# A routed expert stage on one core: ScalarE splits the next expert's weights ahead of a transposing transfer, and second-layer pieces ahead of the rows out

## The reference

```python
logits = x @ w_gate                       # 1792 tokens, 8 experts
e_idx = np.argmax(logits, axis=1)
...
for e in range(E):                        # w1[e] is 768 x 1024, w2[e] is 1024 x 768
    mask = e_idx == e
    ...
    h = np.maximum(x[mask] @ w1[e], 0.0)
    ye = h @ w2[e]
    out[mask] = gate_w[mask, None] * eom[mask, e, None] * ye
```

## Time and profile before

| | |
|---|---|
| median of 3 runs | 1074.93 us (1073.94 to 1076.77) |
| profiled execution | 1075.34 us, span of its trace 1073.5 us |
| PE busy | 1044.1 us, 97% of the span |
| DVE, ACT, POOL busy | 551.5, 422.8, 254.8 us |
| loads issued by SP and ACT for weights, queue q1 | 106.37 MB |
| granted TensorE clock | mean 0.998 of full |

### The profile page before, as it was taken

One profiled execution on the slowest core, in us unless ns is written; L12 is line 12 of the kernel. 1 busy time (PEld: TensorE's weight loads), 2 busy tenths in 40 slices (PEclk: granted clock), 3 DMA queues, 4 the chain that ended last, 5 costly groups with the idle time before them and its releaser, 6 DMA issues. The chain is left out here.

```text
span 1073.5 us, 20362 instructions
## 1 busy us (share of the span) xinstructions
PE 1044.1 (97%) x7916; PEld 608.4 (57%) x7916; DVE 551.5 (51%) x812; ACT 422.8 (39%) x610; POOL 254.8 (24%) x217
## 2 busy tenths in 40 slices
PE   7999999999999999999999999999999999998997
PEld 3434334434555555555555555556777877877775
DVE  7899999984434443333333321003547347256461
ACT  6788888886211111111111221001135335335441
POOL 5887778841000000000000100000112212212221
PEclk9999999999999999999999999999999999999999
DMA  6266877541411111111100432100399388388752
GB/s 159 62 139 138 171 149 158 125 96 36 133 50 51 49 51 55 58 59 59 59 30 1 161 104 74 44 29 30 103 245 297 98 271 274 103 274 262 235 152 48
DMA packets 145832, 125.91 MB, mean 117 GB/s; under 512 B 99825, under 2 KB 121711, under 8 KB 145761
## 3 DMA queue, kind: packets, MB, share of 16 engines
q1 hardware_dynamic: 113952, 106.37, 34.4%
q10 hardware_dynamic: 28640, 7.55, 4.7%
q0 software_dynamic: 3168, 11.02, 2.9%
HBM read 99.49 MB, written 13.85 MB: 106 GB/s over the span
## 5 line engine op out<-in xcount | busy, mean ns | idle before, releaser
L1722 PE MATMUL ps<-arena 128*128 128x448 f16 x1728 | 328.8, 352 | 0.0
L1722 PEld LDWEIGHTS ps<-arena 128*128 128x128 f16 x1728 | 168.2, 98 | 156.1 <-issue 0.5
L1737 PE MATMUL ps<-arena 128*128 128x392 f16 (+1 forms) x996 | 165.3, 329 | 0.0
L1290 DVE SCALAR_TENSOR_TENSOR arena<-arena 128x768 f16<-128x768 f32 (+1 forms) x112 | 112.7, 1067 | 101.3 <-ACT arena L983 100.5
L1801 PE MATMUL ps<-arena 128*128 128x384 f16 x864 | 144.4, 326 | 11.0 <-DVE arena L1510 10.9
L1793 PE MATMUL ps<-arena 128*128 128x128 f16 x2592 | 147.7, 219 | 0.0
L1793 PEld LDWEIGHTS ps<-arena 128*128 128x128 f16 x2592 | 146.2, 98 | 2.4 <-DVE arena L1493 0.2
L1737 PEld LDWEIGHTS ps<-arena 128*128 (+1 forms) x996 | 97.3, 98 | 66.9
L950 ACT ACTIVATE arena<-ps 128x448 f32<-128x448 f32 x48 | 26.1, 543 | 258.2 <-PE ps L1722 258.2
L1618 PE MATMUL ps<-arena 128*128 128x448 f32 x288 | 126.6, 562 | 0.0
L1801 PEld LDWEIGHTS ps<-arena 128*128 128x128 f16 x864 | 83.0, 98 | 67.2 <-DVE arena L1510 14.4
(11 more groups left out here) (183 smaller groups left out, 928.0 us busy)
## 6 DMA issues: line engine op xcount, KB each, us to landing
arena<-in_moe_w SPq DMA_DIRECT2D x48, 512.0 KB, 6.3
arena<-in_moe_w SPq DMA_DIRECT2D x64, 384.0 KB, 4.4
arena<-in_qk SPq DMA_DIRECT2D x23, 448.0 KB, 4.7
y_parts<-arena SPq DMA_DIRECT2D x16, 384.0 KB, 2.3
arena<-sums_inv SPq DMA_DIRECT2D x48, 112.0 KB, 2.9
arena<-in_v SPq DMA_DIRECT2D x24, 192.0 KB, 3.0
arena<-in_moe_w_gate SPq DMA_DIRECT2D x12, 384.0 KB, 4.1
arena<-in_moe_w_val SPq DMA_DIRECT2D x12, 384.0 KB, 5.5
```

Of the source, the lines that this page charges most:

```text
L1290: nc.vector.scalar_tensor_tensor(lo, raw_rows(e, p), S_OP, hi, ALU.mult, ALU.subtract).then_inc(w_lo_ready, 1)
L1722: last = nc.tensor.matmul(ps[:, 2 * (b % 2) + g, 0:S], up_w[s][:, g, c, wl], xt[:, b * KC + c, xl], start=(c == 0 and wl + xl == 0), stop= ...
L1737: last = nc.tensor.matmul(ps[:, 4 + 2 * s + h, 0:cols], gt[:, f, gl, bass.ds(t * 128, 128)], wo[:, f, wl, h, 0:cols], start=(f == 0 and gl ...
```

## The change

ScalarE's program alone is written in another order, inside the tile of the expert stage. In the opener of experts 1 to 7 the first four second-layer pieces are split ahead of `rows_done`, and in the opener of experts 1 to 6 the six pieces of the next expert are split ahead of `move_rows(g + 2)`. Tile 0 and all tiles that are not openers keep their order. No instruction is added or taken away, and no other engine's program changes.

```diff
             def tile(e, s, before, first):
                 g = before + 1
-                if not is_at(g, 0):
+                if is_at(g, 0):
+                    split_high(e, s, range(KC + 5, PIECES))
+                else:
+                    if first:
+                        split_high(e, s, range(KC, KC + 4))
                     rows_done(before)
-                if first:
-                    split_high(e, s, range(KC + 5, PIECES) if is_at(g, 0) else range(KC, KC + 4))
                 hidden(g, 0)
                 if first and not is_at(g, 0):
                     split_high(e, s, range(KC + 4, PIECES))
                 hidden(g, 1)
-                move_rows(g + 2)
+                if is_at(g, 0):
+                    move_rows(2)
                 if first and not is_at(e, E - 1):
                     split_high(e + 1, 1 - s, range(KC))
+                if not is_at(g, 0):
+                    move_rows(g + 2)
```

## The result

| | before | changed |
|---|---|---|
| median | 1074.43 us (4 runs) | 1088.77 us (4 runs, 1083.50 to 1089.43) |
| ratio, 95% interval | | 1.0114 (1.0080 to 1.0149) |
| profiled execution, its span | 1075.34, 1073.5 | 1083.50, 1081.6 |
| TensorE's waits from 790 us on | 10.9 | 16.4 |
| granted clock, mean | 0.998 | 0.993 |

The change made the kernel slower; forecast was 1066.5, so the blind prediction was wrong in sign. Its trace shows the kind of loss, and 8.1 us of it in the span.

The account below looks back on a forecast made before the run. TensorE, busy 97% of the span, was taken as the bound, with 10.9 us of expert-stage waits to win. Of these 8.9 could go, less 0.5: 8.4 off 1075.34 gives 1066.9, set at 1066.5 for the median; range 1064.8 to 1071.0.

Parts of the forecast that it names:

- I take 7.1, the nearest case: Transposing transfer moved behind six splits: 7.1 us from issue to landing beside loads, chosen among 5.9, 7.1 and 10.2.
- Not before its old time: GpSimd's gather of the next expert's opener rows, waiting for the transfer: expected 0.8 to 1.5 us before its old time.
- rival D: Slower, chance 0.08: transfer takes 10.2 us or more beside second-layer loads; four openers wait 2.7 each; 1.9 slower, 1076.8.
- D's point of decision: Transfer time from which the slower outcome, late gathers and waiting openers, was to decide: 9.7 us.
- The rule of packets: Transfer engines alternate between queues packet by packet: adds up to 12.5 us, transfer 15.7, kernel some 1099; held at 0.01.
- The first edit's gain in openers: Rows out behind four splits: VectorE's low half comes 0.8 to 0.9 us earlier; expert 1's opener keeps 0.2 + 0.4.
- The second's in followers: Six splits ahead of the transfer: waits for VectorE in four followers, 4.7 us in all, can go.
- ScalarE's path: ScalarE in followers, from the end of the transfer's issue to the next rows out: 0.6 us.
- the sum: TensorE's 10.9 us of expert-stage waits: 8.9 can go, less 0.5 for near misses, 8.4 gained; forecast 1066.5.

Follow-up runs that it names:

- number 3: Changed kernel, with SyncE holding loads of pieces 7 to 13 of experts 2 to 7 until the preceding opener's transposing transfer lands: 1069.33 us, ratio 0.9946.
- number 6: Changed kernel, loading only 384 of 768 columns of pieces 7 to 13 of experts 2 to 7 (output not the reference's): 1064.34 us, ratio 0.9897.
- number 9: Changed kernel, loading only 576 of 768 columns of pieces 7 to 13 of experts 2 to 7 (output not the reference's): 1069.27 us, ratio 0.9959.
- number 4: Kernel before, rows out still first, but two of the six next-expert splits ahead of the transposing transfer and four behind it: 1078.23 us, ratio 1.0039.
- number 1: Kernel before, with only the rows out moved behind four splits; the transposing transfer stays ahead of the six splits: 1078.57 us, ratio 1.0042.
- number 2: Kernel before, with only the transposing transfer moved behind the six splits; rows out stay first: 1093.49 us, ratio 1.0174.
- number 5: Kernel before, ScalarE's order unchanged, only loads of pieces 7 to 13 of experts 2 to 7 held until the transposing transfer lands: 1083.64 us, ratio 1.0060.
- number 7: Kernel before, two of six splits ahead of the transposing transfer, rows out first, second-layer loads held until that transfer lands: 1076.18 us, ratio 1.0015.

## Why the prediction was wrong

**The step that failed is one term:** "I take 7.1, the nearest case", the transfer's time beside loads. It took 11.7 to 12.7 us in the chain. I had priced it by transfers that ran beside first-layer loads, and hardly beside them: of the 7.1 us only 3.8 had packets of the transfer (1017.7 to 1021.5), with 112 load packets next to them, where expert 4's after had 9.2 us (949.7 to 958.9) and 331. The edit put it behind the six splits, and the low splits are what releases second-layer loads; so the edit both moved the transfer and queued up to six loads of 384 KB beside it. With them held it took 3.7 us, and the kernel 1069.3 (number 3). Numbers 3, 6 and 9 show that it is the load bytes beside it.

**"Not before its old time" became the bound.** I had the next gather at 0.8 to 1.5 us earlier than before, hidden by a few tenths. With 12 instead of 7 us it waited 7 to 10 us for the transfer, as rival D said. D's mechanism, place and direction are what happened; I gave it 0.08, and its price, 1.9 us slower against the 14.3 measured, was too low. It had a wait of 2.7 us in each of four openers; three waited 2.2, 4.1 and 3.8 us, and the fourth, expert 3's, 1.4 behind a stop of 2.5. And it left out that a long wait also slows the matmuls behind it: three groups at 9.65 instead of 7.97, 5.0 us. D's point of decision, 9.7 us of transfer, was about right: number 9's 10.1 us in expert 4 was followed by a wait of 0.28 in expert 5's opener, the changed kernel's 12.1 by one of 2.22.

**The rule of packets** (the Trainium skill, "DMA: Bandwidth & Descriptors", "Queues, rings and completion order") had given 15.7 us. The measured 12.4, and 15.9 in number 4, lie nearer to it than my 7.1. But my 15.7 took one load packet for each packet of the transfer, 1568, and beside expert 4's there were 331. The same section speaks of packets that typically hold some 9 to 17 descriptors, and no run here shows what the profile counts as a packet in these terms. So the nearness of 15.7 is in part luck. That halving the bytes of each load packet at about the same count took the transfer from 12.1 to 7.2 fits turns taken by packets; it doesn't exclude other ways of sharing. I had read two short rows against it, from a place where the queued loads were others.

**What was right.** The first edit's gain in openers: expert 1's waits fell from 1.5 to 0.2 us (0.6 forecast), and they were 0.4 in number 1 and 1.4 in number 2, which lacks this edit. The second's in followers: all four waits for VectorE are gone in the changed kernel. ScalarE's path: 0.5 us between the issue's end and the rows out in expert 4 (946.88 + 2.17 to 949.51), 0.6 forecast. Number 6 shows that with lighter loads the sum held: 1064.3 against 1066.5.

**What else was missed.** That each edit alone costs was not asked: the first one +4 (number 1), the second +19 (number 2). Together they cost 14 by the medians, and under the hold the first is worth 7.7. I had valued it at about 3 us. A part of why is traced above, the share of each part isn't measured.

**Open.** Of six executions of the changed kernel four took 1088.2 to 1089.4 and two, one of them the profiled, 1083.2 and 1083.5; what the four lose beyond that isn't seen. Number 5's loss by the hold is seen at one place only, and why number 7 gained so little is not settled.

## What to carry to other kernels

Before a transfer is moved behind work, ask what that work releases onto the same queues, and price the transfer among those neighbours, not among the ones it had. A buffer of one (`x_rows` here) turns the landing time of one transfer into the start of the next; find the step at which it decides and what it costs beyond the wait. If a reorder fails so, holding back the loads that are not yet needed can save it, but only together with it: the hold alone cost 6 us by its ratio here (9 by the medians), in part because the held loads then ran beside the next gather.

## What the runs showed of the hardware

**The clock after a wait.** Mean granted clock after, in the group behind the 2.2 us wait (973.40 to 983.00), and in an undisturbed one (955.20 to 963.10); columns: stretch, length, busy time and count of PE, PEld, DVE, ACT, POOL, then PEclk, DMA share, GB/s:

```profile
973.40:983.00 9.60, 9.51 (x49) 5.31 (x50) 9.45 (x12) 6.38 (x8) 3.55 (x4) 0.82 0.94 358
```

```profile
955.20:963.10 7.90, 7.90 (x54) 4.79 (x52) 1.68 (x3) 0.60 (x1) 1.08 (x2) 1.00 0.77 168
```

A mean of 0.82 over 9.6 us is some 3.5 us at the lower of the two levels (1.2 GHz), which costs 1.7 us, what the group was longer by. So the three long waits of this execution cost 1.7 us each beyond their length. It is not a matter of the length alone: in number 6 a wait of 2.42 us was followed by a group at 7.97, in number 5 one of 2.66 and in number 4 one of 3.48 by a half group at the usual 4.07.

**Code loads queue too.** TensorE's one wait for nothing but issue, 2.51 us at 877.46, goes with a load of 16 KB of code on queue 8 that was caught among the loads. In 871 to 874 after, and in 869 to 872 before, the columns being packets, MB, share of 16 engines:

```profile
q8 instruction: 1, 0.02, 10.2%
```

```profile
q8 instruction: 1, 0.02, 2.1%
```

One packet at 10.2% of 16 engines over 3 us took 4.9 us, against 1.0. It ran from 871.21 to 876.09, and TensorE went on at 877.46, in the middle of a group. Number 4 has a second such case: a code load from 908.87 to 911.67, and TensorE, stopped within a group, went on at 913.14. That TensorE stood for these loads is read from their coincidence alone.
